# A retention, expert and channel-mixing kernel: batches routed in turn, and the first expert in tiles of 128

## What is computed

```python
logits = np.einsum('bsd,de->bse', x, w_gate)
local_gate = 1.0 / (1.0 + np.exp(-np.einsum('bsd,de->bse', x, w_local).squeeze(-1)))
for b in range(B):
    prev_e = -1
    for s in range(S):
        fresh_e = int(np.argmax(logits[b, s]))
        if s == 0 or local_gate[b, s] < 0.5:
            e = fresh_e
        else:
            e = prev_e if prev_e >= 0 else fresh_e
        prev_e = e
        ...
        h = np.maximum(x[b, s] @ w1[e], 0.0)
        out[b, s] = p[e] * (h @ w2[e])
```

## Time and profile before

| | us |
|---|---|
| median of 3 runs | 476.57 (473.64 to 476.89) |
| the profiled execution | 472.91 |
| its span, first to last instruction | 471.2 |
| TensorE busy | 443.1 (94%) |
| VectorE busy | 262.9 (56%) |
| ScalarE busy | 193.5 (41%) |
| GpSimd busy | 98.5 (21%) |

### The profile page before, as it was taken

How to read it: one execution, slowest core, us unless ns; L and a number is a source line. 1 busy time by engine, 2 the same in 40 slices (tenths; PEclk the granted TensorE clock), 3 DMA queues, 4 the chain that set the end, 5 groups by cost and what they waited for, 6 DMA issues and landing times.

```text
span 471.2 us, 8138 instructions
## 1 busy us (share of the span) xinstructions
PE 443.1 (94%) x2895; PEld 399.4 (85%) x2896; DVE 262.9 (56%) x421; ACT 193.5 (41%) x306; POOL 98.5 (21%) x102
## 2 busy tenths in 40 slices
PE   7799998579999999999999992899999999999997
PEld 7798897578989898989898981898899889889985
DVE  2676895673757474747484834885154454615401
ACT  1134332063636363635353632886245344624400
POOL 2535760410414141415151511000000000000000
PEclk9899999799999999999999996899999999999999
DMA  6999983153475747565659413500100010010001
GB/s 220 405 400 332 320 336 113 45 176 140 172 275 171 275 170 278 190 263 189 264 162 379 134 45 103 187 1 0 46 24 0 22 45 0 0 45 22 1 22 45
DMA packets 28476, 70.88 MB, mean 150 GB/s; under 512 B 3170, under 2 KB 4194, under 8 KB 28452
## 3 DMA queue, kind: packets, MB, share of 16 engines
q1 hardware_dynamic: 22946, 57.95, 33.8%
q0 software_dynamic: 2816, 9.18, 5.3%
q10 hardware_dynamic: 2690, 3.44, 2.0%
HBM read 59.79 MB, written 10.76 MB: 150 GB/s over the span
## 4 chain that ended last, share of the span: by engine, by line
PE 89%; DMA 4%; DVE 2%; issue 2%; POOL 1%; ACT 1%; SPq 0%; POOLq 0%; DVEq 0%; ACTq 0%
PE bank L1036 25%; PE bank L1038 24%; PE bank L1037 24%; PE bank L965 3%; PE bank L954 3%; PE bank L941 2%; PE bank L975 2%; PE bank L983 2%; PE bank L1047 2%; PE bank L990 1%; DMA decay<-powers_dram 1%; DMA keep<-y_dram 1%; DMA x_tok<-x_dram,slots 1%; POOL slot_col L420 1%; DMA powers_dram<-pw 1%
## 5 line engine op out<-in xcount | busy, mean ns | idle before, releaser
L1036 PE MATMUL bank<-xh,wh 128*128 128x256 f32 x256 | 72.5, 283 | 2.4 <-issue 2.4
L804 DVE TENSOR_TENSOR wl<-raw,wh 128x1024 fp32r<-128x1024 f32 x64 | 73.4, 1218 | 1.9 <-ACT wh L506 1.9
L1038 PE MATMUL bank<-xh,wl 128*128 128x256 f32 x256 | 72.4, 283 | 0.0
L1037 PE MATMUL bank<-xl,wh 128*128 128x256 f32 x256 | 72.4, 283 | 0.0
L506 ACT ACTIVATE wh<-raw 128x1024 fp32r<-128x1024 f32 x64 | 61.7, 1052 | 2.2 <-issue 1.5
L1036 PEld LDWEIGHTS bank<-xh,wh 128*128 128x128 f32 x256 | 49.1, 192 | 3.0 <-issue 2.7
L1036 PE MATMUL bank<-wh,hh 128*128 128x512 f32 x128 | 50.6, 396 | 0.0
L1037 PE MATMUL bank<-wl,hh 128*128 128x512 f32 x128 | 49.9, 390 | 0.0
L1038 PE MATMUL bank<-wh,hl 128*128 128x512 f32 x128 | 49.9, 390 | 0.0
L1037 PEld LDWEIGHTS bank<-xl,wh 128*128 128x128 f32 x256 | 49.1, 192 | 0.3
L1038 PEld LDWEIGHTS bank<-xh,wl 128*128 128x128 f32 x256 | 49.1, 192 | 0.0
(11 more groups left out here) (161 smaller groups left out, 852.4 us busy)
## 6 DMA issues: line engine op xcount, KB each, us to landing
raw<-in_w_dram SPq DMA_DIRECT2D x64, 512.0 KB, 6.1
qk_sb<-in_qk_dram SPq DMA_DIRECT2D x12, 512.0 KB, 7.2
kv_sb<-in_kv_dram SPq DMA_DIRECT2D x12, 512.0 KB, 5.9
x_dram<-keep ACTq DMA_DIRECT2D x12, 256.0 KB, 6.4
keep<-y_dram SPq DMA_DIRECT2D x12, 256.0 KB, 4.4
out_dram<-o_sb SPq DMA_DIRECT2D x12, 256.0 KB, 2.0
raw<-in_w_k_dram SPq DMA_DIRECT2D x4, 512.0 KB, 10.6
raw<-in_w_v_dram SPq DMA_DIRECT2D x4, 512.0 KB, 7.8
```

The source lines that it names most:

```text
L804: dve.tensor_tensor(parts[1 - p][1][:, c, :], raw[:, c, :], parts[1 - p][0][:, c, :].bitcast(F32), ALU.subtract).then_inc(s["part_l"], 1)
L1036: pe.matmul(ps, lhsT=a_high, rhs=b_high, start=start, stop=False)
L1037: pe.matmul(ps, lhsT=a_high, rhs=b_low, start=False, stop=False)
L1038: return pe.matmul(ps, lhsT=a_low, rhs=b_high, start=False, stop=stop)
```

## The change

- Routing is done for each batch by itself. That of batch 0 runs inside the attention loop: its codes at the end of iteration 6 on VectorE, the running maximum in 7, the choice in 8, the places in 9, the tables at the end of 9 and the slots in 10; TensorE's small products for it stand at the head of iterations 7 to 10. VectorE makes both tables alone.
- Expert 0 is done in tiles of 128 tokens, with products of 128 columns in the first layer. Its first tile holds tokens of batch 0 alone (padded to 128 at least). GpSimd gathers it in iteration 10, ahead of its last `first_low`; TensorE transposes it after iteration 11. The products of the routing of batch 1 stand between the first-layer products of that tile, at fixed places (`CODE_AT` and so on). The other tiles of expert 0 (tile 1 to `own` - 1, `own` from the plan) go through a loop of their own, which also transposes the first unit of expert 1.
- The other seven experts go in units of 256 as before, in a loop of two experts to a turn; the weights of the outputs and the exponential come later, in the first tile. The `keep_warm` transposes after the attention loop are gone. `x_dram` and `y_dram` have the 128 spare rows between the batches.

The core of the diff:

```diff
+    CODE_AT, RUN_AT, PLACE_AT, SLOTS_AT, FETCHED_AT = 5, 8, 14, 27, 4
...
+        def own_tiles(eng):
+            return eng.value_load(plan[0:1, 0:1], min_val=2, max_val=TILES_MAX)
...
+                if t == NC + 4:
+                    for x in y_out:
+                        pool.wait_ge(x, 16)
+                    pool.wait_ge(x_stored[0], 16 * NC)
+                    pool.wait_ge(s["x_slots0_done"], 1)
+                    pool.indirect_dma_start(out=xs_tok[0], out_offset=None, in_=x_dram[0:S + P, :],
+                                            in_offset=bass.IndirectOffsetOnAxis(ap=x_slots0[:, 0:1], axis=0)).then_inc(s["xs_in"], 16)
...
+            fetch_tile(slots[:, 1:2])
+            fetch(slots[:, NT:NT + 2])
+            pool.wait_ge(s["ys_done"], 1)
+            scatter_tile(0, x_slots0[:, 0:1])
...
+            own = own_tiles(pool)
+            with pool.Fori(1, own) as i:
+                pool.wait_ge(s["xs_ps"], i + 1)
+                pool.tensor_copy(xs_slots[:, :], slots[:, bass.ds(i + 1, 1)]).then_inc(s["xs_slots_done"], 1)
+                pool.wait_ge(s["xs_slots_done"], i)
+                pool.sem_inc(s["pool_passed"], 1)
+                fetch_tile(xs_slots[:, 0:1])
...
+            for f in range(4):
+                hs_high(0, f)
+                for c in range(2 * f, min(2 * f + 2, CH - CH_LATE)):
+                    weights_high(0, c)
+            act.wait_ge(s["exp_in"], 1)
+            act.activation(expd[:, :, :], shifted[:, :, :], ACT.Exp).then_inc(s["exp_done"], 1)
+            xs_high(1, 1)
...
+            def route_code(b):
+
+                lg = whole(logits, b)[:, :, 0:E]
+                dve.wait_ge(s["logits_done"], FIRST + (b + 1) * NC)
+                link(dve.tensor_reduce(whole(mx, b), lg, AX_X, ALU.max))
+                link(dve.tensor_tensor(cand[:, :, :], lg, whole(mx, b).unsqueeze(2).to_broadcast([P, NC, E]), ALU.is_equal))
+                dve.scalar_tensor_tensor(out=fresh[:, 0:NC], in0=whole(logits, b)[:, :, E:E + 1].rearrange("p n o -> p (n o)"), scalar=0.0,
+                                         in1=whole(first, b), op0=ALU.is_lt, op1=ALU.max)
+                link(dve.scalar_tensor_tensor(out=cand[:, :, :], in0=cand[:, :, :], scalar=-float(E), in1=iota_tok[:, :, :],
+                                              op0=ALU.mult, op1=ALU.add))
+                link(dve.tensor_reduce(whole(code, b), cand[:, :, :], AX_X, ALU.min))
+                dve.tensor_tensor(whole(code, b), whole(code, b), fresh[:, 0:NC], ALU.mult).then_inc(s["code_done"], 1)
+
...
+            def route_tables(b):
+                dve.tensor_tensor(slot_row[:, :, :], iota_row[:, :].unsqueeze(1).to_broadcast([P, NC, P]),
+                                  whole(row, b).unsqueeze(2).to_broadcast([P, NC, P]), ALU.is_equal).then_inc(s["tables_done"], 1)
+                dve.wait_ge(s["value_done"], b + 1)
+                for n in range(NC):
+                    t = b * NC + n
+                    dve.tensor_scalar(slot_col[:, n, :], iota_row[:, 0:COLS], col[:, t:t + 1], value[:, t:t + 1],
+                                      ALU.is_equal, ALU.mult).then_inc(s["tables_done"], 1)
...
+                if t == NC + 1:
+                    route_run(0)
+                if t == NC + 2:
+                    route_choose(0)
+                if t == NC + 3:
+                    route_place(0)
+                if t == NC + 4:
+                    first_slots()
...
+                    route_code(0)
+                if t == NC + 3:
+                    route_tables(0)
+            xs_low(0, 0)
...
+            route_code(1)
+            route_run(1)
+            route_choose(1)
+            hs_low(0, 0)
+            route_place(1)
+            route_tables(1)
+            hs_low(0, 1)
+            hs_low(0, 2)
+            dve.wait_ge(s["slots_ps"], 2)
+            dve.wait_ge(s["x_slots0_done"], 2)
+            dve.tensor_tensor(slots[:, :], route_ps[1][5], slots0[:, :], ALU.add).then_inc(s["slots_done"], 1)
+            hs_low(0, 3)
...
+            xs_low(1, 1)
+            dve.wait_ge(s["ys_ps"], 1)
+            dve.wait_ge(x_stored[1], 16 * NC)
+            dve.tensor_copy(y_sb[0], psO[:, :]).then_inc(s["ys_done"], 1)
...
+                dve.wait_ge(s["ys_ps"], i + 1)
+                dve.wait_ge(s["ys_out"], i * 16)
+                dve.tensor_copy(y_sb[1], psU[:, :]).then_inc(s["ys_done"], 1)
+                xs_low(i + 1, 1)
+            for c in range(CH - CH_LATE, CH):
+                weights_low(0, 0, c)
...
+                if t == NC:
+                    pe.wait_ge(s["run_done"], 1)
+                if t == NC + 1:
+                    pe.wait_ge(s["onehot_done"], 1)
+                if t == NC + 2:
+                    pe.wait_ge(s["ahead_done"], 1)
+                if t == NC + 3:
+                    pe.wait_ge(s["x_slots0_done"], 2)
...
+                if NC < t <= NC + 4:
+                    pe.wait_ge(s["logits_done"], FIRST + t - 1)
+                if t == NC + 1:
+                    code_rows(0)
+                if t == NC + 2:
+                    run_columns(0)
+                if t == NC + 3:
+                    places(0)
+                if t == NC + 4:
+                    slot_rows(0)
...
+            def hs_product(a, p, f, i, c):
+                cols = slice((2 * f + i) * P, (2 * f + i + 1) * P)
+                return three_products(psH[f][:, i * P:(i + 1) * P], [w[:, c, cols] for w in w1p[p]], [xsh[a][:, c, :], xsl[a][:, c, :]],
+                                      start=(c == 0), stop=(c == KD - 1))
...
+            pe.wait_ge(s["first_l"], CH)
+            pe.wait_ge(s["xsl_done"], 1)
+            group = 0
+            for f in range(4):
+                for i in range(2):
+                    for c in range(KD):
+                        if group == CODE_AT:
+                            code_rows(1)
+                        if group == RUN_AT:
+                            run_columns(1)
+                        if group == PLACE_AT:
+                            places(1)
+                        if group == SLOTS_AT:
+                            slot_rows(1)
+                        mm = hs_product(0, 0, f, i, c)
+                        group += 1
+                mm.then_inc(s["hs_ps"], 1)
+            for f in range(KF):
+                if f % 2 == 0:
+                    pe.wait_ge(s["hsl_done"], f // 2 + 1)
+                if f == FETCHED_AT:
+                    pe.wait_ge(s["keep_done"], FIRST + NT)
+                    tile_transposes(1, 1, psX)
+                mm = ys_product(0, f)
+            mm.then_inc(s["ys_ps"], 1)
...
+            own = own_tiles(pe)
+            with pe.Fori(1, own) as i:
+                pe.wait_ge(s["xsl_done"], i + 1)
...
+                mm.then_inc(s["ys_ps"], 1)
+                pe.wait_ge(s["x0l_done"], i * 2 + 2)
+                pe.sem_inc(s["pe_passed"], 1)
+                tile_transposes(i + 1, 1, psX)
...
+            pe.wait_ge(s["x0l_done"], own * 2)
+            pe.wait_ge(s["xsl_done"], own + 1)
+            pe.wait_ge(s["ys_done"], own)
+            pe.sem_inc(s["pe_passed"], 1)
+            with pe.Fori(0, E // 2 - 1) as ep:
+                lo, hi = plan_of(pe, ep * 2 + 1)
+                expert(ep * 2 + 1, 1, lo, hi)
+                expert(ep * 2 + 2, 0, hi, plan_ahead(pe, ep * 2 + 2))
```

More of the change, by code:

```diff
@@ L215, in mixer_kernel @@
         x_in = [sem(f"s_x_in{i}") for i in range(2)]
+        x_stored = [sem(f"s_x_stored{b}") for b in range(B)]
         y_out = [sem(f"s_y_out{i}") for i in range(2)]
@@ new lines, in route_place @@
+            def route_place(b):
+                _, _, _, place, count, _ = route_ps[b]
+                dve.wait_ge(s["place_ps"], 2 * b + 2)
+                link(dve.tensor_tensor(flat(placed_in[:, :, :]), place, onehot[b][:, :], ALU.mult))
+                with nc.allow_low_precision(reason="ranks are whole numbers that a float holds exactly"):
+                    link(dve.tensor_reduce(whole(rank, b), flat(placed_in[:, :, :]).rearrange("p (e n) -> p n e", e=E), AX_X, ALU.add))
+                link(dve.tensor_single_scalar(whole(over, b), whole(rank, b), 7, ALU.arith_shift_right))
+                dve.scalar_tensor_tensor(out=whole(row, b), in0=whole(over, b), scalar=-float(P), in1=whole(rank, b),
+                                         op0=ALU.mult, op1=ALU.add).then_inc(s["row_done"], 1)
+                dve.wait_ge(s["rank_done"], b + 1)
+                dve.tensor_tensor(whole(col, b), whole(over, b), whole(colbase, b), ALU.add).then_inc(s["row_done"], 1)
+                dve.wait_ge(s["row_done"], 2 * b + 2)
+                dve.tensor_tensor(whole(value, b), whole(back, b), whole(row, b), ALU.subtract).then_inc(s["value_done"], 1)
+                if b == 0:
+                    dve.tensor_tensor(ahead[:, :], count[0:1, :], floor[:, :], ALU.max).then_inc(s["ahead_done"], 1)
@@ L742, in _ @@
```

(21 more changed lines are left out.)

438 lines of the change are left out of this document (256 added, 182 removed).

## The result

The changed kernel takes 488.03 us (median of 4 runs, 486.78 to 489.66) against 476.71 of the kernel before on the same chip: ratio 1.026, interval 1.0215 to 1.0305. It is 2.6% slower. The forecast was 477.0 with a range of 469 to 485.5, so the time lies outside, 2.5 us above its upper end.

What follows compares the result with a forecast made beforehand. TensorE was taken to bound almost everything, except one 21 us hole. Filling it was offset by a 5 us longer loop, a second weight pass and a seam of 3: 121.1 against 120.9, +0.2, so 477 us, range 469 to 485.5.

Steps and rivals of the forecast that it cites:

- Part 2: First tile and second batch's routing: first product at 81.9, spacing 0.107, fetch stall 0.7, tile done at 100.0.
- clock 1.00 throughout: Sign of a right forecast: TensorE's granted clock never falls; a 0.50 row between 50 and 125 counts as wrong.
- Part 1: First batch's routing inside the attention loop: VectorE's added small instructions make the loop 5 us longer.
- a choice between 3.0 and 7.1: Loop loss in us: 3.0 if no small VectorE operation waits for GpSimd, 7.1 if each does; 5 taken.
- the layout: Instruction-by-instruction schedule of the attention loop; largest loss put in iteration 10, TensorE waiting 1.5 to 2.2 for the last table.
- Part 3: Second tile 17.0 us, ending at 117.0, then the seam and emptied queues; second expert's first product at 121.1.
- 1.08: Seam before the second expert: us for TensorE to load registers and enter the expert loop before its first product.
- Long waits let the clock fall: Slower rival: waits in iterations 7, 10 and the seam halve the clock; +7.5 us, 484; chance 0.18.
- The counter-argument: Against the half-clock rival: each TensorE wait is shorter than the idle stretch where the clock fell before.
- The other rivals: Narrow products as plain f32: 508, chance 0.08; spacing following columns: 470.3, faster 0.22; a third tile: 494, 0.02.
- The signs named ahead: Wrong if second expert starts outside 116 to 126, clock 0.50 between 50 and 125, spacing outside 0.09 to 0.13, or unit gaps.

Runs made afterwards that it cites:

- e_warm_loop: Changed kernel with spare transposes (8, 8 and 12) before TensorE's waits in attention-loop iterations 8, 9 and 10; 486.12 us, ratio 1.0241 to the kernel before.
- e_before_tail: Kernel before the change, with 80 spare transposes added behind the last unit; 475.60 us, ratio 1.0013 to the kernel before.

## Why the prediction was wrong

**The step that failed** is the size of the first tile in Part 2, 18.1 us (81.9 to 100.0), which rested on "clock 1.00 throughout". It took 26.6. Its working was good at 2.4 GHz: a spacing of 0.107 forecast, 0.111 measured; no stall for the second tile's fetch; 19.6 less 1.0 = 18.6 for the tile when the clock held, 0.5 over the forecast. But 17 us of it ran at 1.2 GHz, and I had looked for falls only where TensorE waits. That is 8.5 of the 12.4 us by which the second expert started later than forecast (133.48 against 121.1).

**Part 1** forecast 5 us for the longer loop. The last logits came 9.0 later (83.81 against 74.86, 8.95); less 1.2 for the start and 2.7 for the fall at 70.8 that is 5.0. That it is the 5 of the forecast is in part luck: 5 was a choice between 3.0 and 7.1, and the time was not lost where the layout put it. Iterations 7, 8 and 9 became 0.8, 1.2 and 1.5 us longer, iteration 10, which was to be the largest piece, only 1.1 without its fall, and the first tile's transposes, which now stand ahead of the last logits, are 0.4 of the sum. The clock on top of it was not counted: 2.7 us, and 1.2 at the start that may be chance. The Trainium skill's lock (SBUF — State Buffer, "SBUF: two separate sides") holds in the rows of L814 and L827: small operations wait their turn, against the end of 3.0. L813 and L826, which have one tensor input, waited as well (1.32 and 1.20 against 0.17). The Trainium skill names there, beside two-input operations, those in a 2-port perf mode, and these two may be such; no run here shows their mode. The forecast spoke of two inputs alone. The Trainium skill's 81 ns for 128 columns (TensorE: Matmul & The Clock Gate, "Back-to-back issue gap") did not hold for these four-byte products, 0.111 and so 37% more.

**Part 3.** The second tile took 17.65 (forecast 17.0). From its end to the second expert 3.7 against 4.1 forecast, which held 1 us for restarts elsewhere. 1.08 was too little for the registers: VectorE's low copy ends at 131.13 and the product starts at 133.48, 2.35 later.

**The rivals.** "Long waits let the clock fall" was the right mechanism for two of the three falls, held at 0.18. Of its three places iteration 10 and the seam came true, at 2.7 and 2.5 where it priced 2.6; iteration 7 did not. The fall in iteration 10 began at its very start (70.8), ahead of that iteration's own wait and behind waits in 8 and 9, which the rival did not name. What it lacked is the costliest fall, in a tile without a wait. The counter-argument, that each wait is shorter than the idle stretch of the kernel before, did not bear: in the loop three gaps of 0.67, 0.57 and 1.04 us, 7 to 10 us apart, stood ahead of the fall, and with the last two filled (e_warm_loop) it did not come. The other rivals fell: the spacing was neither 0.067 nor 0.272, and two tiles ran. The range failed because no case had a fall outside a wait; with 8.0 more the rival's 484 would have been 492, and the truth lay between.

**The signs named ahead** did their work: a clock row of 0.50 between 50 and 125 and a start outside 116 to 126 were both to count as wrong, and both are there.

## What to carry to other kernels

When a change fills a hole on a TensorE-bound path, look at how dense the new work is and not only at its length: narrow products mixed with tiny matmuls can run at half clock although TensorE counts as busy for the whole stretch, and half the columns then cost more than all of them (26.6 against 19.6 us). Price each seam with one fall (here 2.5 us for a wait of 3.7) until a profile shows that there is none, and try the cheap cures first: wider products, a few spare ones, register loads ahead of the wait. Small VectorE work put beside long GpSimd operations can cost what is left of GpSimd's operation (1.0 to 1.3 us here), not its own 0.2. And take more than one profile of each kernel before a difference of a few us is put on a bill.

## What the runs showed that I had not expected

- Doubling the columns of 96 products made the kernel 6.1 us faster (488.25 to 482.11).
- The same code can fall at other times. The loop and routing of e_before_tail are those of the kernel before; its profile has 0.50 from 78.3 to 95.4 where the first had 85.6 to 92.3, and its last y copy starts at 289.69 and not at 284.52. So two executions of one kernel can stand 5 us apart, for the most part by the clock's falls, and the spread of the 29 runs of the kernel before is 6.9.
- One-input int32 operations of 128x6 took 1.32 and 1.20 us beside GpSimd and 0.17 without it.
